# Sorted rows without gaps, plain loads for the feed-forward, and indirect stores for the final rows, in a kernel of attention, experts and feed-forward

## What is computed

```python
# attention, per batch and head, over 768 steps t
S = a_n[t][:, None] * S + outer(k[t], v[t])      # complex a_n, |a_n| at most 0.999
y[t] = q[t] @ real(S)
# x: the 3072 tokens, 8 heads x 48 = 384 wide
e_idx = argmax(x @ w_gate, axis=1)
gate_w = softmax(x @ w_gate)[e_idx]
eom = sigmoid(x @ w_output_gate)[e_idx]
out[tok] = gate_w * eom * (relu(x[tok] @ w1[e]) @ w2[e])      # e = e_idx[tok], w1 384 x 1024
# feed-forward on the result
h = out @ w_in                                    # 384 x 2048
return maximum(0.01 * h, h) @ w_out
```

## Time and profile before

| | us |
|---|---|
| median of three runs | 1136.29 |
| lowest and highest | 1134.42, 1142.38 |
| profiled execution, its own time | 1135.07 |
| its span in the profile | 1133.3 |
| PE busy in the span | 967.5 (85%) |
| POOL, ACT, DVE busy | 494.1, 438.7, 430.1 |

### The profile page before, as it was taken

One profiled execution on the slowest core, in us unless ns is written; L12 is line 12 of the kernel. 1 busy time (PEld: TensorE's weight loads), 2 busy tenths in 40 slices (PEclk: granted clock), 3 DMA queues, 4 the chain that ended last, 5 costly groups with the idle time before them and its releaser, 6 DMA issues. The chain is left out here.

```text
span 1133.3 us, 17921 instructions
## 1 busy us (share of the span) xinstructions
PE 967.5 (85%) x5874; PEld 849.7 (75%) x5875; DVE 430.1 (38%) x670; ACT 438.7 (39%) x660; POOL 494.1 (44%) x339
## 2 busy tenths in 40 slices
PE   0249888989997019999999998799999999999998
PEld 0037776777786018999989987699999999999998
DVE  3467767767763602333332322222221222222111
ACT  6767767766531202222222211233333333333322
POOL 0244443444331573743577397424324343343322
PEclk9999888889999559999999999799999999999999
DMA  5223233223220734323434252100001010010000
GB/s 210 72 72 115 59 119 114 78 82 86 76 78 2 271 132 146 113 99 135 153 104 146 93 206 97 57 1 23 34 0 56 0 56 0 0 56 0 29 1 28
DMA packets 48679, 90.56 MB, mean 80 GB/s; under 512 B 23144, under 2 KB 39680, under 8 KB 45056
## 3 DMA queue, kind: packets, MB, share of 16 engines
q1 hardware_dynamic: 43264, 55.46, 15.1%
q0 software_dynamic: 5376, 34.61, 8.8%
HBM read 65.99 MB, written 24.02 MB: 79 GB/s over the span
## 5 line engine op out<-in xcount | busy, mean ns | idle before, releaser
L1397 POOL TENSOR_TENSOR act_r<-act_f,act_r 128x512 fp32r<-128x512 f32 x96 | 124.7, 1299 | 258.1 <-ACT act_r L1442 258.1
L1520 PE MATMUL bank<-x,w_in_r 128*128 (+1 forms) x864 | 219.4, 399 | 1.2 <-DVE x L1475 1.2
L1533 PE MATMUL bank<-w_out_r,act_r 128*128 128x384 f32 x1152 | 217.4, 337 | 0.0
L1533 PEld LDWEIGHTS bank<-w_out_r,act_r 128*128 128x128 f32 x1152 | 204.8, 188 | 8.2
L1520 PEld LDWEIGHTS bank<-x,w_in_r 128*128 128x128 f32 x864 | 161.6, 190 | 31.6 <-DVE x L1475 1.6
L1481 DVE TENSOR_TENSOR act_f<-bank,small 128x512 f32<-128x512 f32 x96 | 66.5, 692 | 284.1 <-ACT small L1439 277.1
L1274 PE MATMUL bank<-wm,x_tr 128*128 x522 | 128.4, 400 | 3.9 <-POOL wm L1178 1.6
L1439 ACT ACTIVATE small<-bank 128x512 f32<-128x512 f32 x96 | 57.5, 599 | 188.3 <-PE bank L1520 186.1
L1296 PE MATMUL bank<-wm,h_tr 128*128 x696 | 128.6, 339 | 1.6 <-DVE h_tr L1232 1.6
L1296 PEld LDWEIGHTS bank<-wm,h_tr 128*128 128x128 f32 x696 | 120.1, 188 | 1.9 <-issue 1.9
L1274 PEld LDWEIGHTS bank<-wm,x_tr 128*128 128x128 f32 x522 | 96.8, 190 | 24.8 <-issue 5.0
(11 more groups left out here) (171 smaller groups left out, 1408.4 us busy)
## 6 DMA issues: line engine op xcount, KB each, us to landing
stage<-moe_w POOLq DMA_DIRECT2D x12, 1536.0 KB, 6.9
qkv_in<-in_qkv SPq DMA_DIRECT2D x24, 576.0 KB, 5.7
a_in<-in_a SPq DMA_DIRECT2D x8, 1152.0 KB, 6.0
x_sorted<-zeros SPq DMA_DIRECT2D x8, 816.0 KB
stage<-moe_w SPq DMA_DIRECT2D x4, 1536.0 KB, 8.1
x_b<-x_sorted SPq DMA_DIRECT2D x31, 192.0 KB, 2.5
y_sorted<-y_b SPq DMA_DIRECT2D x29, 192.0 KB, 1.9
out<-o_sb SPq DMA_DIRECT2D x24, 192.0 KB, 1.9
```

The lines of the kernel that those rows point to most:

```text
L1397: pool.tensor_tensor(a[:, 1, :], act_f[f % 2][:, :], a[:, 0, :].bitcast(F32), ALU.subtract).then_inc(s_gl, 1)
L1520: last = pe.matmul(h_bank[f % 2][:, :], w_in_r[:, wp, t * F2 + f * P:t * F2 + (f + 1) * P], x2[:, xp, bass.ds((w % 2) * (KT * XW) + t * XW ...
L1533: last = pe.matmul(o_bank[j][:, 0:W], a[:, ap, j * P:(j + 1) * P], w_out_r[:, wp, f * W:(f + 1) * W], start=(f == 0 and n == 0), stop=(f = ...
```

## The change

- `x_sorted` has no gaps: expert e's rows follow directly on those of e - 1. A block still starts at its expert's next 128 rows; the last block of an expert reads and stores some rows of the next one too, and the next one's block overwrites them. The table has one more number per block, its first row, and SP reads it for every load and store. The eight clears in the attention and the one of `y_sorted` go; 256 rows behind the last are cleared at the start of the route.
- A row of `x_sorted` has 386 columns: the 384, the token's gate value, and the token's number. So the gate is worked out before the positions, and DVE multiplies a loaded block by it (`gated`, L1372 of the changed kernel) before PE transposes it. The scaling in the feed-forward goes.
- `stage` holds two quarters of 1536 columns instead of two halves of 3072, and POOL splits and loads the weights in quarters.
- Experts and feed-forward are one program without a barrier between them. The feed-forward takes the rows in sorted order, by plain loads of SP (`window`); those of window 0 are issued when all but the last two blocks are stored, and their transposes stand in PE's code for the last block. The windows are written out instead of looped over.
- At a window's end POOL scatters the four output tiles by the tokens' numbers (`ids`, read from the 386th column), with indexed stores.

Cut to its core:

```diff
 # experts: SP
-            def load(g):
-                sp.dma_start(x_b[:, :], xs[bass.ds(g * P, P), :]).then_inc(s_xb, 16)
+            def load(g):
+                row = at(sp, T_ROW, g, 0, N)
+                sp.dma_start(x_b[:, :], xs[bass.ds(row, P), :]).then_inc(s_xb, 16)
             def store(g):
                 sp.wait_ge(s_y, g + 1)
-                sp.dma_start(ys[bass.ds(g * P, P), :], y_b[:, :]).then_inc(s_ys, 16)
+                row = at(sp, T_ROW, g, 0, N)
+                sp.dma_start(ys[bass.ds(row, P), :], y_b[:, :]).then_inc(s_ys, 16)
+            def window(w):
+                for j in range(TW):
+                    need(sp, s_tt, TW * (w - 1) + j + 1)
+                    t = TW * w + j
+                    sp.dma_start(xg[j][:, :], ys[t * P:(t + 1) * P, :]).then_inc(s_in[j], 16)
             load(0)
-            for g in range(1, 3):
-                sp.wait_ge(s_tx, g)
-                load(g)
-            with sp.Fori(0, last_g) as g:
-                sp.wait_ge(s_tx, g + 3)
-                load(g + 3)
-                store(g)
-            store(last_g)
+            sp.wait_ge(s_tx, 1)
+            load(1)
+            last_g = last_block(sp)
+            sp.wait_ge(s_tx, 2)
+            load(2)
+            store(0)
+            before = at(sp, T_LAST, 1, N // P - 2, NBMAX - 2)
+            with sp.Fori(1, before) as g:
+                sp.wait_ge(s_tx, g + 2)
+                load(g + 2)
+                store(g)
+            sp.wait_ge(s_ys, before * 16)
+            window(0)
+            sp.wait_ge(s_tx, last_g + 1)
+            load(last_g + 1)
+            store(before)
+            store(last_g)
+            sp.wait_ge(s_ys, last_g * 16 + 16)
+            window(1)
+            sp.dma_start(ids[:, :].unsqueeze(2),
+                         xs[0:N, W + 1:W + 2].bitcast(I32).rearrange("(t p) a -> p t a", p=P),
+                         allow_slow_non_contiguous=True).then_inc(s_ids, 16)
+            for w in range(2, NW):
+                window(w)
 # experts: DVE
+            def gated(g):
+                dve.wait_ge(s_xb, 16 * g + 16)
+                dve.tensor_scalar(x_b[:, 0:W], x_b[:, 0:W], x_b[:, W:W + 1], None, ALU.mult).then_inc(s_xg, 1)
             with dve.Fori(1, last_g) as g:
+                gated(g + 2)
                 trailing(g)
                 block_tokens(g + 2)
                 result(g)
 # POOL: weights, now in quarters
-                half = stage[:, i * WE:(i + 1) * WE]
+                part = stage[:, u % 2 * QE:(u % 2 + 1) * QE]
 # PE: the seam
-            transpose_hidden(last_g)
-            layer2(last_g)
-            pe.wait_ge(s_ys, last_g * 16 + 16)
-            pe.wait_ge(s_xb, last_g * 16 + 48)
+            for j in range(2):
+                transpose_token(0, j)
+            transpose_hidden(last_g)
+            for j in range(2, TW):
+                transpose_token(0, j)
+            layer2(last_g)
+            pe.wait_ge(s_wq, 4 * (E + 2))
+            pe.wait_ge(s_xl, last_g + 2)
+            ff1(0, 0)
+            pe.wait_ge(s_y, last_g + 1)
+            ff1(0, 1)
 # feed-forward: POOL
-                if more:
-                    gather(w + 1, True)
-                for f in range(FT2):
-                    ...
+                for f in range(2, FT2):
+                    trail(w, f)
+                if more:
+                    for f in range(2):
+                        trail(w + 1, f)
+                scatter(w)
+            for f in range(2):
+                trail(0, f)
+            pool.wait_ge(s_ids, 16)
 # attention: SP
-                if unit(i, 2):
-                    lot = TB * P // UNITS
-                    clear(xs[bass.ds((i - 2) * lot, lot), :], LOT_P, lot // LOT_P)
 # route: DVE, ahead of the counts
+            dve.wait_ge(s_e, 2)
+            step(dve.tensor_reduce(den[:, :], te(soft), AX_X, ALU.add))
+            ...
+            dve.tensor_tensor(x_all[:, :, W:W + 1], gate[:, :].unsqueeze(2), den[:, :].unsqueeze(2),
+                              ALU.mult).then_inc(s_pos, 1)
```

More of the change, by code:

```diff
@@ new lines, in _, with experts_then_feed_forward, late @@
+            sp.dma_start(xs[N:N + 2 * P, :].rearrange("(p r) w -> p r w", p=P),
+                         zeros[:, :].unsqueeze(1).to_broadcast([P, 2, XR])).then_inc(s_fill, 16)
+            for u in range(6):
+                if u >= 2:
+                    sp.wait_ge(s_wq, u - 1)
+                sp.dma_start(stage[:, u % 2 * QE:(u % 2 + 1) * QE],
+                             moe_w[u // 4][:, u % 4 * QE:(u % 4 + 1) * QE]).then_inc(s_stage[u % 2], 16)
+            sp.wait_ge(s_fill, 16)
+def experts_then_feed_forward(nc, ctx, sem, sb, bank, ident, ids, table, stage, masks_at, wm, wbase, w_out_r, ys,
+                              moe_w, w_in, w_out, xs, out, s_stage, s_wq):
+    T_ROW, T_SLOT, T_READY, T_CUM, T_LAST = 0, TB, 2 * TB, 3 * TB, 3 * TB + E
+    WE = KT * F1
+    QE = WE // 2
+    HF = FT1 // 2
+    XW = TW * P
+    w_in_r = nc.alloc_sbuf_tensor_at("w_in_r", [P, 2, KT * F2], F32R, offset=wbase)
+    place = [wbase + 4 * 4 * WE]
+    def late(name, shape, dt=F32):
+        t = nc.alloc_sbuf_tensor_at(name, shape, dt, offset=place[0])
+        place[0] += (4 * math.prod(shape[1:]) + 31) // 32 * 32
+        return t
+    x_b = nc.alloc_sbuf_tensor_at("x_b", [P, XR], F32, offset=masks_at)
@@ L1320, in feed_forward @@
[L1320 to L1350 removed]
+    s_ids = sem("token_ids_in")
@@ new lines, in quarter @@
+            def quarter(pair, q):
+                return pair.rearrange("p a n -> p (a n)")[:, q * QE:(q + 1) * QE]
+            for e in range(1, E):
+                done = at(pool, T_CUM, e - 2, 1, NBMAX) if e >= 2 else None
+                for q in range(4):
+                    split(e, q, quarter(wm[:, e % 2, 0:2, :], q), quarter(wm[:, e % 2, 2:4, :], q), done)
+            for q in range(4):
+                split(E, q, w_out_r[:, 0, q * QE:(q + 1) * QE], w_out_r[:, 1, q * QE:(q + 1) * QE], None)
@@ L1492, in body @@
                         hidden(FT2 * (w + 1) + f, f)
-            for j in range(TW):
-                scale(0, j)
-            for j in range(TW):
+            gated(0)
+            block_tokens(0)
+            gated(1)
+            block_tokens(1)
+            gated(2)
+            trailing(0)
+            block_tokens(2)
+            result(0)
+            with dve.Fori(1, last_g) as g:
+                gated(g + 2)
+                trailing(g)
+                block_tokens(g + 2)
+                result(g)
+            for j in range(2):
                 tokens(0, j)
+            trailing(last_g)
+            for j in range(2, TW):
+                tokens(0, j)
+            result(last_g)
             for f in range(2):
```

571 lines of the change are left out of this document (253 added, 318 removed).

## The result

The changed kernel takes 1248.0 us (median of 4 runs, 1238.34 to 1251.54), the kernel before beside it 1136.64 (4 runs): a ratio of 1.096 (95% interval 1.088 to 1.103), so 111 us slower. Direction and place were forecast; of the size, 66 of 111 us were, and 1248 lies 3 us above the range of 1153 to 1245. The profiled execution took 1251.54 us, span 1249.8, 116.5 more than the span before.

What follows compares the result with a forecast made beforehand. The matmul engine was taken to bound the expert stage (busy 257.38 of 259 us). Terms 69 + 5 + 2 - 15.6 + 2.2 - 2 + 0.5 + 5 = +66 gave a median of 1202 us, range 1153 to 1245.

Steps and rivals of the forecast that it cites:

- The load behind the store: Expert loop: x_b's load after the store and two row reads starts layer 2 late, 1.85 us per iteration.
- The gate multiplication beside GpSimd: Expert loop: VectorE's gate multiplication waits for GpSimd's weight split, 0.7 us per block.
- The clock falls in the new gaps: Rival, chance 0.13: TensorE's gaps in the expert loop lower its clock, +54 us if in every block, 1256.
- half of them: Milder form of the clock rival: lower clock in half of the expert blocks, 1229 us.
- The last iteration and the start: Expert stage: iteration 27 +5 us for its late load and token loads; first gate multiplication at the start +2.
- The seam: Experts to feed-forward: the 13.6 us gap goes and full clock saves 2.9, transposes cost 1.0: -15.6 us.
- w_in would be late only in a faster loop: Seam: w_in's 12 quarters take 70 us, against seven blocks of 67 at the old period, 84 at the new.
- the quarters bind: Part of the rival that loads are in time (chance 0.12): weight quarters then come late, +5 us.
- Route: Route: the gate's steps come ahead of the positions, less waits and block arithmetic that go: net +2.2 us.
- Attention: Attention: eight clears of 816 KB go, -2 us, with 0 and -12 as ends.
- The ids: Feed-forward: token ids must land before the third subtraction of window 0, +0.5 us (0 to 5).
- Tail: End of kernel: four indexed stores and GpSimd's drain after the last copies, +5 us (3 to 6).

Runs made afterwards that it cites:

- run 1: Changed kernel with SyncE's x_b load issued before the store again, all else kept: 1146.99 us, 1.010 of the kernel before.
- run 2: Changed kernel with the gate multiplication moved from VectorE to ScalarE, the load still behind the store: 1223.13 us.
- run 4: Changed kernel with both the x_b load before the store and the gate multiplication on ScalarE: 1144.56 us.
- run 6: Kernel of run 4, layer 1 of an expert's first block waiting for two quarters only: 1137.87 us; with window 0's loads and ids also earlier: 1137.15 us.
- run 7: Second kernel of run 6 with w_in ahead of half of w_out in GpSimd's list: 1130.23 us, 0.9952 of the kernel before.
- run 5: Changed kernel with useless matmuls added between layer 1 and the transposes of x_b: six per block 1221.50 us, twelve 1205.59 us.

## Why the prediction was right and wrong

**The load behind the store: right.** I had written T0 + 7.1 for layer 2; the trace has T0 + 7.3 in undisturbed blocks. The two row reads are 1.92 (I took 1.9), which is luck in part: I had 0.95 for each, and they are 0.64 and 1.28. The landing is 2.4 (2.5), and run 1 shows that the order alone brings 101 of 111 us back. 2.04 per block instead of 1.85: 5 us.

**The gate multiplication beside GpSimd: right in kind, too large in size.** The 0.7 per block were to be 19 us; the long multiplications are 12: six took over 2.1, a seventh 1.40. I had reckoned with the rest of the long operation, 1.7 in the mean; the six met the short one. What I had no term for is the transfer of x_b behind a transfer of weights, another 13 us. I had the maximum of 5.2 for x_b's landing in the earlier trace rows and used it only for the upper end. A load issued at T0 + 3.5 has no room for it, one issued at T0 + 5.7 in the block before has.

**The step that failed** is the lower clock, which the sum put at nothing: "*The clock falls in the new gaps*" stood beside it as a rival of 0.13, with "*block gaps are short, and layer 1 is hidden under the wait*" against it. It happened in 20 of 27 blocks and is 37 us, most of what the sum lacked (44 in the loop, 50 in all). Its price I had right: 2.0 for a block at the lower level, measured 1.8 in the mean. But I set it up as another way for things to go, where it follows from my own case: I had forecast 1.8 to 3 us of standstill per block and had a row in which such a stretch ran at 0.75. It belonged in the sum: with 27 more (that rival's "half of them") the sum's 1202 is 1229, with 54 it is 1256; 1248 lies between. The Trainium skill (TensorE: Matmul & The Clock Gate, "Why this matters for your kernels") warns of gaps above about 3 us. In the changed kernel the fall came with the waits of 2.3 to 4.3 us and in the block behind, as the rival's own "*the longer waits behind GpSimd*" had it; run 2 shows it behind regular gaps of 1.3 to 1.5 us too, and there the measurement decides.

**The last iteration and the start: right.** Iteration 27 took 17.7, 8.2 over the old period (2.55 + 5 forecast); the start +2.4 (2).

**The seam: right.** -13.6 and -2.9 against -15.6 in all. That w_in would be late only in a faster loop was right as well, and so was the rival's "*the quarters bind*" (runs 1, 4, 6), though its 5 us were 11 in the loop and 6 to 8 at the seam.

**Route: right**, 2.2. **Attention: -2 forecast, no gain seen**: two traces with the clears end at 362.66 and 365.22, ten without them at 364.0 to 366.4, so 2 us could not have been told apart. **The ids: right**: GpSimd waited 2.9 us for them and TensorE not at all. **Tail: +8 for +5**: issue and landing came as set out (the last lands 2.6 after its start), but the drain behind them takes 4.80, not the 2.02 of the route's.

So 101 of the 111 us hang on the order of load and store in SyncE's loop, and the rest on weights that come late. The change's own gain, 16.5 us at the seam, was real; put right (runs 6 and 7) the kernel keeps 5 to 6 of it, after route (2) and tail (8) above all.

## What to carry to other kernels

When a load moves behind a wait, ask not only whether it still arrives in the mean, but whether it has room for its longest landing, and what large transfer was issued a microsecond before it. A gap that you forecast on TensorE has a second price, the lower clock in the matmuls behind it: put it into the sum with the gap, not beside it. The same operation need not cost the same at each place: a register load in front of the store took 0.27 us, the same one behind the store's issue 0.55. A fault that dominates covers others: here the slow loop hid weights that come 4 to 6 us late, and each repair showed the next.

## What the runs showed of the hardware

- Two short gaps (1.3 to 1.5 and 0.4 us) in each block came with the lower clock in 14 of 25 blocks (run 2). In the changed kernel 12 useless matmuls of 0.19 us per block brought full clock back in 26 of 27 (run 5): more work, 42 us less time.
- What waits for x_b (193 KB) started 2.2 to 2.5 us after the load's issue as a rule, 4.9 to 5.2 after it when 768 KB had been issued 0.8 to 1.1 us earlier, and 6.8 behind 1.5 MB issued 0.86 us earlier.
- A VectorE multiplication of 0.42 took up to 2.2 beside a GpSimd operation of 1.5, and up to 3.4 beside a subtraction of 3.5 (run 1); with two inputs in SBUF (0.56) up to 3.6. It ended 0.2 to 0.4 us after the operation in its way. On ScalarE (0.61) it was never longer (run 2).
- A register load on SyncE took 0.27 us, and 0.54 to 0.67 in the loop of the changed kernel when it stood right behind the issue of a store.
- GpSimd's drain took 4.80 us at the end of the program, behind four indexed stores, and 2.03 at the end of the route, behind 24 of them.
